# DFT and two MLPs on one Trainium2 core: rows of batches 1 to 3 transformed beside the MLP, tables split by parity of s, tiles of 502 columns

## What is computed

```python
def _attn_ref(x):                       # x: 4 x 3008 x 256
    X = np.fft.fft(x, axis=1)
    X = np.fft.fft(X, axis=2)
    return X.real
def _moe_ref(x, w_in, w_out):           # w_in 256 x 2048, w_out 2048 x 256
    r = np.maximum(x @ w_in, 0.0)
    return (r * r) @ w_out
def _moe2_ref(x, w_in, w_out):
    h = x @ w_in
    return (h * np.cos(h)) @ w_out
reference = _moe2_ref(_moe_ref(_attn_ref(x)))   # on the 12032 rows
```

## Time and profile before

| what | value |
|---|---|
| median of the timed runs | 2050.89 us |
| profiled execution, its own time | 2050.13 us |
| its span, first to last instruction | 2048.3 us |
| busy: PE, DVE, ACT | 1969.3 (96%), 1429.9 (70%), 1279.4 us (62%) |
| mean granted TensorE clock | 0.987 of full speed |
| VectorE's first MLP instruction | 158.66 us after the start |
| VectorE's first instruction of up item 15 of tile 0 | 243.88 us |
| matmuls | 8662, of them 8064 of 504 and 486 of 378 columns |

### The profile page before, as it was taken

One profiled execution on the slowest core, in us unless ns is written; L12 is line 12 of the kernel. 1 busy time (PEld: TensorE's weight loads), 2 busy tenths in 40 slices (PEclk: granted clock), 3 DMA queues, 4 the chain that ended last, 5 costly groups with the idle time before them and its releaser, 6 DMA issues.

```text
span 2048.3 us, 21425 instructions
## 1 busy us (share of the span) xinstructions
PE 1969.3 (96%) x8662; PEld 1629.5 (80%) x8662; DVE 1429.9 (70%) x1529; ACT 1279.4 (62%) x1297; POOL 0.2 (0%) x4
## 2 busy tenths in 40 slices
PE   5786899999999999999999999999999999999998
PEld 5785778888888888888888888888888888888887
DVE  6945667677667677677677677677677667667665
ACT  3345667667667667657657657657657657657655
POOL 0000000000000000000000000000000000000000
PEclk9899999999999999999999999999999999999999
DMA  5642000000000000000000000000000000000000
GB/s 191 223 150 85 11 16 11 16 11 11 16 11 11 16 11 11 16 11 11 16 11 11 15 11 11 16 10 11 16 11 11 16 11 11 0 11 11 1 11 21
DMA packets 21579, 55.20 MB, mean 27 GB/s; under 512 B 1892, under 2 KB 12644, under 8 KB 19944
## 3 DMA queue, kind: packets, MB, share of 16 engines
q1 hardware_dynamic: 18272, 47.61, 6.8%
q10 hardware_dynamic: 3208, 6.22, 0.8%
HBM read 35.22 MB, written 18.60 MB: 26 GB/s over the span
## 4 chain that ended last, share of the span: by engine, by line
PE 88%; DVE 5%; ACT 4%; DMA 2%; issue 1%; SPq 0%; ACTq 0%; DVEq 0%
PE ps L685 88%; DMA xin<-x 1%; ACT u L467 1%; ACT u L472 1%; DVE kbuf L647 1%; DVE u L652 1%; DVE u L653 1%; DVE col L524 1%; ACT osb L438 1%; DMA wst<-w1o 0%; ACT gh L471 0%; DVE wo L565 0%; DMA tin<-tables 0%; DVE wi L565 0%; DVE tab L503 0%
## 5 line engine op out<-in xcount | busy, mean ns | idle before, releaser
L685 PE MATMUL ps<-gh,wo 128*128 128x504 f32 x4608 | 1121.5, 392 | 30.2 <-DVE gh L621 22.3
L685 PEld LDWEIGHTS ps<-gh,wo 128*128 128x128 f32 x4608 | 866.6, 188 | 224.9 <-DVE gh L621 27.4
L685 PE MATMUL ps<-y,wi 128*128 128x504 f32 x2304 | 557.3, 391 | 3.0 <-DVE u L672 1.9
L685 PEld LDWEIGHTS ps<-y,wi 128*128 128x128 f32 x2304 | 433.7, 188 | 95.7 <-DVE u L672 2.4
L657 DVE TENSOR_TENSOR u<-kbuf,ps 128x1008 f32<-128x1008 int32 x192 | 231.2, 1204 | 350.2 <-ACT kbuf L476 350.2
L621 DVE TENSOR_TENSOR gh<-u,gh 128x1008 fp32r<-128x1008 f32 x384 | 461.1, 1201 | 3.3 <-ACT u L472 2.1
L476 ACT ACTIVATE kbuf<-ps 128x1008 int32<-128x1008 f32 x192 | 194.4, 1013 | 357.1 <-PE ps L685 357.1
L467 ACT ACTIVATE u<-u 128x1008 f32<-128x1008 f32 x192 | 201.6, 1050 | 194.8 <-DVE u L653 193.8
L685 PE MATMUL ps<-eo,weo 128*128 128x504 f32 x1152 | 295.7, 392 | 0.9 <-DVE u L653 0.9
L647 DVE SCALAR_TENSOR_TENSOR kbuf<-ab,w,ps 128x504 f32<-128x504 f32 x192 | 141.7, 738 | 181.2 <-PE ps L685 181.2
L685 PEld LDWEIGHTS ps<-eo,weo 128*128 128x128 f32 x1152 | 217.7, 189 | 48.2 <-DVE u L653 1.3
(11 more groups left out here) (44 smaller groups left out, 302.9 us busy)
## 6 DMA issues: line engine op xcount, KB each, us to landing
xin<-x SPq DMA_DIRECT2D x12, 1028.0 KB, 6.5
out<-osb SPq DMA_DIRECT2D x24, 504.0 KB, 2.8
scratch_eo<-est ACTq DMA_DIRECT2D x8, 756.0 KB, 4.1
raw<-scratch_eo SPq DMA_DIRECT2D x12, 504.0 KB, 3.2
tin<-tables SPq DMA_DIRECT2D x12, 378.0 KB, 5.2
ab<-scratch_a SPq DMA_DIRECT2D x12, 252.0 KB, 3.7
wst<-w1i SPq DMA_DIRECT2D x4, 512.0 KB, 5.6
wst<-w1o SPq DMA_DIRECT2D x8, 256.0 KB, 3.1
```

The costliest lines, as they stand in the source:

```text
L685: op = pe.matmul(out_, a, b, start=start and i == 0, stop=stop and i == len(todo) - 1)
```

## The change

- **Tables by parity of s.** Rows s are sorted into even and odd s. All products, of even and of odd k, are now KT x 2 steps of three passes of 378 columns into two halves of a bank (one for each parity of s), 18 matmuls each; 18 products make 324 matmuls. The sum of the two halves gives one half of the rows, their difference the mirrored half: ScalarE copies the odd half (`copy_odd_rows`), VectorE adds and subtracts (`take_rows`, two instructions of 377 columns or fewer, the second waiting for the first). The row sums go through one buffer `est`, whose next use waits for the store before (`est_st`). The data for column 128 comes ready from the host (`x128`).
- **What stays in the front.** Products 0 (column 128, even k), 1 and 2 (batch 0, even k, both phases), folding of batch 0, splitting of the even table (6 pieces of 756 columns) and `w1_product`. Then tile 0 starts.
- **Inside tile 0.** Products 3, 4 and 5 (odd k of batch 0 and of column 128) become `row` items behind up items 6, 12 and 13; they use an `hb` bank. The odd table (12 pieces of 378 columns) and the weights are split there: before it 2 weights, in each of up items 0 to 11 one table piece and one weight, in up items 12 to 15 and in mix items 0 to 5 one weight. There are four stage buffers (six for w2o). Both tables' halves are stored to HBM (`store_tables`, two DMAs of 2.32 MB each time): the even ones behind load 9, the odd ones behind load 27.
- **Inside tiles 1 to 4, 6 and 7** (`MADE_IN`). Each makes one phase of batches 1 to 3. In up(t) and mix(t-1, 1) six pieces of x (512 KB) are loaded and folded, each over four items (`rows_fold`, steps 0 to 3, of 512, 256, 2 x 128 and 256 columns; step 3 is the split, with `rows_high` on ScalarE). In mix(t, 0), items 2 to 4, TensorE makes the product for even k and in items 5 to 7 the one for odd k, two steps (6 matmuls) in each item, behind the item's `down` (`later_rows`), in bank `yb[0]`. The tables come back from HBM in pieces of 387 KB through three buffers (`ring`). The even rows are taken in item 5, the odd ones in up item 0 of the next tile.
- **Tiles** have 502 columns, and `ab`, `osb` and `est` one buffer instead of two; `osb`'s next use waits for the store before.

```diff
-T = 504
-TB = 2 * KP // T
+KP = H // 2 + 1
+T = 502
+TB = 3
...
+PRODUCTS = [(None, 0, 0), (0, 0, 0), (0, 1, 0), (0, 0, 1), (0, 1, 1), (None, 0, 1)]
+PRODUCTS += [(b, phase, odd) for b in range(1, B) for phase in range(2) for odd in range(2)]
+EARLY, INSIDE = 3, 6
+ROW_ITEMS = {6: 3, 12: 4, 13: 5}
+
+MADE_IN = {1: (1, 0), 2: (1, 1), 3: (2, 0), 4: (2, 1), 6: (3, 0), 7: (3, 1)}
...
+def split_order():
+
+
+    weights = ([("o1", p) for p in range(8)] + [("i2", half * WQ + q) for q in range(WQ) for half in range(2)] +
+               [("o2", p) for p in range(8)])
+    order, until = weights[0:2], []
+    for i in range(NF + NM):
+        if i < 4 * KT:
+            order.append(("odd", i))
+        order += weights[i + 2:i + 3]
+        until.append(len(order))
+    return order, until
...
+    def fold_step(it):
+        if it.kind == "up" and it.t in MADE_IN:
+            t, j = it.t, it.index
+        elif it.kind == "mix" and it.sign == 1 and it.t + 1 in MADE_IN:
+            t, j = it.t + 1, NF + it.index
+        else:
+            return None
...
+    def row_pieces(it):
+        if it.kind == "mix" and it.sign == 0 and it.t in MADE_IN and it.index >= 2:
+            b, phase = MADE_IN[it.t]
+            odd = it.index >= 5
+            first = 2 * (it.index - (5 if odd else 2))
+            return number[b, phase, int(odd)], range(first, first + 2)
+        return None
+    def row_taken(it):
+        if it.kind == "row":
+            return it.r
+        if it.kind == "mix" and it.sign == 0 and it.t in MADE_IN and it.index == 5:
+            return number[(*MADE_IN[it.t], 0)]
+        if it.kind == "up" and it.t - 1 in MADE_IN and it.index == 0:
+            return number[(*MADE_IN[it.t - 1], 1)]
+        return None
...
+        def store_tables(odd):
+            if odd:
+                sp.wait_ge(split_lo, order.index(("odd", 4 * KT - 1)) + 1)
+            else:
+                sp.wait_ge(te_lo, 2 * KT)
+            for half in range(2):
+                sp.dma_start(scratch_t[odd, half], tab[odd][half][:, :, :, :].bitcast(F32)).then_inc(tab_st[odd], 16)
...
+        store_rows(3)
+        for n in range(19, O2):
+            load_split(n)
+        store_tables(1)
+        for n in range(O2, O2 + 6):
+            load_split(n)
+        store_rows(4)
+        store_rows(5)
+        sp.wait_ge(est0_st, 16)
+        load_raw(1)
...
+        def copy_odd_rows(r):
+            src, to, rows = row_sums(r)
+            n = columns_of(PRODUCTS[r][2])[0]
+            if r < INSIDE:
                 act.wait_ge(rows_done, r + 1)
+            else:
+                act.wait_ge(ring_used, 6 * (r - INSIDE + 1))
+            if r >= EARLY:
+                act.wait_ge(est_st, 16 * (stores_until(r) - 1))
+            act.activation(to[:, n:2 * n if n > KP - n else KP], src[0:rows, 1, 0:KP - KP // 2],
+                           ACT.Copy).then_inc(odd_copied, 1)
...
+            if row_taken(it) is not None:
+                copy_odd_rows(row_taken(it))
+            if fold_step(it) is not None:
+                n, b, phase, piece, step = fold_step(it)
+                if step == 3:
+                    rows_high(n, piece // 2, piece % 2)
+            for n in splits_in(it):
+                if order[n] == ("i2", 0):
+                    act.wait_ge(tab_st[0], 32)
+                if n == O2:
+                    act.wait_ge(rows_done, INSIDE)
+                    act.wait_ge(tab_st[1], 32)
+                split_high(n)
...
+        def take_rows(r):
+            src, to, rows = row_sums(r)
+            b, phase, odd = PRODUCTS[r]
+            n, mirrored = columns_of(odd)
+            dve.wait_ge(odd_copied, r + 1)
+            dve.tensor_tensor(to[:, 0:n], src[0:rows, 0, 0:n], to[:, n:2 * n], ALU.add).then_inc(plus_done, 1)
+            dve.wait_ge(plus_done, r + 1)
+            even_part, odd_part = src[0:rows, 0, 0:mirrored], to[:, n:KP]
+            if phase:
+                dve.tensor_tensor(odd_part, odd_part, even_part, ALU.subtract).then_inc(rows_out, 1)
+            else:
+                dve.tensor_tensor(odd_part, even_part, odd_part, ALU.subtract).then_inc(rows_out, 1)
...
+        def rows_fold(n, b, phase, kt, parity, step):
+            if step == 0:
+                dve.wait_ge(x_in, 16 * (n + 1))
...
+                dve.tensor_tensor(fold[:, :, :], xin[:, :, 0, :], xin[:, :, 1, :], signs[phase][0]).then_inc(summed, 1)
+            elif step == 1:
+                dve.wait_ge(summed, n + 1)
+                dve.tensor_tensor(fold[:, 0:2, :], fold[:, 0:2, :], fold[:, 2:4, :], signs[phase][0]).then_inc(paired, 1)
+            elif step == 2:
+                dve.wait_ge(paired, n + 1)
+                dve.tensor_tensor(fold[:, 2, :], fold[:, 0, :], fold[:, 1, :], signs[phase][1])
+                dve.tensor_tensor(fold[:, 3, :], fold[:, 0, :], fold[:, 1, :], signs[phase][2]).then_inc(folded, 1)
+            else:
+                dve.wait_ge(fold_hi, n + 1)
+                dve.tensor_tensor(f[0][1][:, kt, parity, :, :], fold[:, 2:4, :],
+                                  f[0][0][:, kt, parity, :, :].bitcast(F32), ALU.subtract).then_inc(fold_lo, 1)
...
+            if row_taken(it) is not None:
+                take_rows(row_taken(it))
+            if fold_step(it) is not None:
+                n, b, phase, piece, step = fold_step(it)
+                rows_fold(n, b, phase, piece // 2, piece % 2, step)
+            for n in splits_in(it):
+                split_low(n)
...
+        def later_rows(r, pieces):
+            first = 6 * (r - INSIDE)
+            if pieces.start == 0:
+                b, phase, odd = PRODUCTS[r]
+                t = next(t for t in made if MADE_IN[t] == (b, phase))
+                if odd == 0:
+                    pe.wait_ge(fold_lo, 3 * (r - INSIDE) + 6)
+                    pe.wait_ge(y2_out, 2 * t)
+                else:
+                    pe.wait_ge(rows_out, r)
+            for i in pieces:
+                n = first + i
+                pe.wait_ge(ring_in[n % 3], 16 * (n // 3 + 1))
+                op = row_step(r, i // 2, i % 2, lambda j: ring[:, n % 3, j, :])
+                op.then_inc(ring_used, 1)
...
+            if row_pieces(it) is not None:
+                later_rows(*row_pieces(it))
```

## The result

| | before | after |
|---|---|---|
| median of the timed runs | 2051.0 us | 2104.67 us |
| span of the profiled execution | 2048.3 us | 2102.6 us |
| VectorE's first k | 158.66 us | 77.37 us |
| from there to k of up item 15 | 85.2 us | 110.15 us |
| from there to the end | 1804.4 us | 1915.1 us |

The ratio is 1.0268, with a 95% interval of 1.0243 to 1.0294: the kernel is 54 us slower. I had predicted 2074 us in a range up to 2104. The sign was right; the size was missed by 31 us, and the time lies just outside the range.

A forecast was written before the change was run, and what follows sets the result against it. TensorE was taken to bound the kernel from about 250 us on. 92.7 us less in the front, 24.4 more in the first tile, 92.2 more after it and 1.8 around the span gave 2074 us, range 2035 to 2104.

The forecast's parts named there:

- first k: Front: VectorE's first k at 66 us instead of 158.66, including 15 us of waits, mostly for weight products and their copies.
- first tile: From first k to k of item 15: 99.1 us of items, 3.5 of row adds, 7 of store stall; 109.6 us.
- columns: From item 15 on: 7800 matmuls each lose 2 of 504 columns, 0.9 ns each, 7.0 us less.
- products in the mix: Mix items: 12 products of 18 matmuls at 0.173 us, all on TensorE, 37.4 us more.
- even before odd: Mix item 5: the odd product waits for the even rows to be taken, 3.2 us six times, 19 us more.
- odd rows in up item 0: Up item 0: row copy and adds delay k of item 1, 3.0 us four times and 2.5 twice, 17 us more.
- fold step 3: Up items 3, 7 and 11 of six tiles: the fold's split delays the next k, 1.0 us 18 times, 18 us more.
- clock: After the 12 stalls of 2 to 3.2 us: low clock about two times in five, 1.2 us each, 5 us more.
- smaller: Split in item 15 +1.3, eo of tile 1 split in mix item 7 +1.0, tile 3's load behind a store +0.5 us.
- Rivals 1 and 2: From item 15 on: all waits and clock absorbed, 2015 us (0.14); or odd-row and step-3 waits only, 2039 us (0.12).
- Rival 4: x or the ring arrives late, TensorE waits for DMA in six tiles: 108 us, 2182 us in all; chance 0.03.
- Rival 3: First tile: slow table stores at 200 GB/s, stall of 18 instead of 7 us, 2090 us in all; chance 0.11.

The follow-up runs named there:

- the run with the even product before the odd one: Changed kernel with each odd product's 12 pieces made in mix items 6 and 7, none in item 5: 2083.23 us, ratio 1.0167.
- the run with 502 columns: Kernel before, rows 2016 bytes apart, computing only the first 502 of 504 columns in tiles after the first: 154.39 us a tile, ratio 1.0017.
- The fillers: Changed kernel with unused matmuls of 512 columns put before the second, third and fourth weight products of the front: 2100.22 us, ratio 1.0248.
- the one with rows of 2016 bytes: Changed kernel, still 502 columns, with rows of y1, gh and eo 2016 bytes apart instead of 2008: 2105.92 us, ratio 1.0282.

## Why the prediction was wrong

Profiled span 2102.6 us against the 2072.2 of my sum, step by step:

| step | predicted | measured | off by |
|---|---|---|---|
| first k | 66 us | 77.37 | +11.4 |
| first tile | 109.6 us | 110.15 | +0.5 |
| columns | -7.0 us | 12 x 0.47 = +5.6 | +12.6 |
| products in the mix | +37.4 us | 6 x 6.04 = +36.2 | -1.2 |
| even before odd | 6 x 3.2 = +19 | 6 x 3.22 = +19.3 | +0.3 |
| odd rows in up item 0 | 4 x 3.0 + 2 x 2.5 = +17 | 4 x 3.55 + 2 x 2.83 = +19.9 | +2.9 |
| fold step 3 | 18 x 1.0 = +18 | 18 x 1.1 = +19.8 | +1.8 |
| clock | +5 us | +9.1 | +4.1 |
| smaller | +2.8 us | about +1 | -2 |

(measured: the spacing of k in tiles with the step less that in tiles without it, at full clock, the products as in the run with the even product before the odd one; the clock is what the slow ones of the same kind took more; "smaller" is what is left of the 110.7 us.)

**Right: the mechanism of the waits and the first tile.** The waits were in the places named, and each was worth its price when taken out: 21, 16 and 19 us with the clock that hangs on them, against 19, 18 and 17. The first tile is right by its terms: 6.68 to 6.75 us an item against 6.69, 6.32 against 6.27 with one weight, and 7.2 us of stall against 7. Rivals 1 and 2 (absorbed waits) are out: of the waits forecast, none was given back. Rival 4 is out as well; the list of TensorE's waits shows none for `ring` or x. Rival 3 would have shown in a first tile of 120 us; by its own numbers its stall is 34 - 13.5 = 20.5 us and not 18.

**Wrong: "Columns: 7800 matmuls lose 2 of 504 columns, 0.9 ns each."** I divided a measured time by its columns and took the quotient for the price of one. The trace of before had matmuls of one length only in this regime, so nothing in it bore that out. The term was -7.0 us and measured +5.6. It needed bounds like the other unknown costs, with no gain and a loss among them. And I didn't look at what else 502 changes: the rows of gh, y1 and eo move from 2016 to 2008 bytes. By the Trainium skill ("TensorE: Matmul & The Clock Gate", "Back-to-back issue gap") the gap between isolated matmuls is N / 2.4 GHz plus 2.5 ns, which would make two columns 0.8 ns, by an estimate from it; the run with 502 columns, a stream of matmuls and 0.19 us a tile slower, doesn't show that.

**Wrong: the front's "waits 15".** The duration of a product was taken from its 12 long matmuls at the low clock, 4.71 us, without the 16 of two columns before them, 3.57 us at that clock. In the new order ScalarE and VectorE wait for each product in turn, so VectorE waits 24.4 us there and not 14. The fillers give back 6.0 of these 10.4 us, which are clock; the other 4.4 are not taken apart. The last 1.0 us of the 11.4 is the start: VectorE's first split of w1 is at 9.78 us and not at 8.76.

**Too small: the clock.** I priced 12 gaps at two of five and 1.2 us. Six of 12 had it, at 1.3 to 1.8 us; a seventh, in tile 4 (the 4.70 us above), is low too, but its time is in part that of the wait for the output bank, and it is in the table under the odd rows. What I quoted beside it from the Trainium skill ("TensorE: Matmul & The Clock Gate", "HAM oscillation"), that the clock falls each time, is said there of waits of 3 to 5 us. For these gaps of 2.3 to 3.0 us it would have given too much in this execution (12 x 1.5 = 18 us), but not by far in the one with rows of 2016 bytes (nine of 12, 16 us).

**The range.** It was built from whole rivals, and had no room for several terms off in one direction. Rivals 1 and 2 took most of its width on the side where the time wasn't.

## What to carry to other kernels

Where an engine pair works as a chain and TensorE takes its turns from it, the place of a small step decides its price: row adds of 1.1 us cost 2.8 to 3.6 us at the end of an item and 0.3 us at its head, ahead of the wait for TensorE. Before shrinking a tile by a few columns, look at what the new size does to the distance of rows in SBUF, and take the gain as zero until one run shows it. When an engine waits in turn for small pieces of TensorE's work, count every matmul of a piece, the short ones too, at the clock that TensorE has behind the gap. Moving work under the bound engine paid here only when no gap opened with it: the same moved products made the kernel 2.7% slower with their gaps and, with three steps reordered, 0.5% faster.

## What the runs showed of the hardware

- With 504 columns in rows 2016 bytes apart a tile of 672 matmuls takes 154.20 us, in rows 2024 bytes apart 154.53; with 502 columns 154.21 to 154.39 and, 2008 bytes apart, 154.67.
- The gain from 504 to 480 columns is 6.48 us a tile, from 504 to 496 it is 1.5, from 504 to 502 none.
- The stretch from 45 to 49 us, with TensorE busy for 3.94 of 4.00 us and 16 of its 17 matmuls two columns wide, has a granted clock of 0.50. 16 such matmuls take 3.57 us there, and 1.84 to 2.10 us behind wide ones.
- Whether a gap of 2 to 3 us is followed by the low clock differs between gaps of the same kind in one execution; it cost 1.3 to 1.8 us in six of the 12 in the changed kernel.
